# The opening block of a linear-attention and two-layer feed-forward kernel: the diagonal of y by products of its own, and another order of its queues

## The chip, the cores and the metric

The kernel runs on one core of one Trainium2 chip. The metric is device time in microseconds (us) for one execution, lower is better; a run's time is given as the median of several executions.

## The reference, cut to what matters

Four batches, eight heads, 768 tokens, 48 values a head. A linear attention with decay runs first, and two feed-forward layers follow it on the 3072 tokens.

```python
for t in range(S):                     # r, k, v: (4, 8, 768, 48), w, u: (8, 48)
    cur = einsum('bhd,bhe->bhde', u * k[t], v[t])
    y[t] = einsum('bhd,bhde->bhe', r[t], state + cur)
    state = w * state + einsum('bhd,bhe->bhde', k[t], v[t])
x = y as (B * S, H * D)                # 3072 x 384
x = relu(x @ w_in) ** 2 @ w_out        # 384 -> 2048 -> 384
x = (x @ w_a) * (x @ w_b) @ w_out2     # 384 -> 1536 -> 384
```

The term `cur` makes the diagonal: token t sees itself through sum over d of r, u and k, times v[t]. Everything earlier comes through the scores within a block of 64 tokens and through the state.

## The kernel before

**Tiles.** The tokens are cut into six blocks of 512, and a block into four units of 128 columns. A unit e holds 64 tokens of two batches (i = 0, 1), with the heads in pairs (g) of two (q). Per unit the attention does this: TensorE transposes k and r into PSUM (`turn_k`, `turn_r`), VectorE multiplies them with tables of powers of w into `kT` and `rT` (`scale_k`, `scale_r`), TensorE makes the scores (`score`, 32 small matmuls), VectorE copies the entries of earlier tokens into the `scores` tile through the mask `earlier` (`mask`), GpSimd and VectorE make the diagonal numbers `diag` (`k_times_u`, `times_r`, `sum_diagonal`), TensorE makes y from the state and the scores (`mix_state`, `mix_scores`) and the state's new part (`renew_state`), ScalarE copies y out (`take_y`) and VectorE the state (`keep_state`).

Before, the `scores` tile is first filled with a matrix that is zero apart from `diag` on its diagonal, and `mask` writes the rest over it. In the first block that matrix is made by eight ScalarE activations for units 0 and 2 (`make_diagonals`), by one VectorE multiplication for unit 1 (L1268) and by one GpSimd multiplication for unit 3 (L570).

**The feed-forward part.** Each product is made of three passes (hi x hi, hi x lo, lo x hi) over float32 split into two parts: `split_hi` (ScalarE, L383) and `split_lo` (VectorE, L389) split a tile of weights once; the token matrix `xT` is split as well. `up(n, f)` and `down(n, f)` are the first layer's step f in block n, 9 and 9 matmuls of 512 columns; `up2` and `down2` are the second layer's. The attention of block n + 1 is laid beside the steps of block n by the table `beside`.

**The opening.** Only the first block's attention has nothing to stand beside. It is written out by hand on each queue, and every queue runs strictly in the order written. `up(0, 0)` (L723) waits for all four units of x (`x_lo_made` 4). Units 0 and 1 get there through DMAs: `take_y` writes `y_pad`, `repack` on SyncE (SP, L359 and L361, six DMAs) brings it into `xT` rows, then `x_hi` (ScalarE, L935) and `x_lo` (VectorE, L1206). Units 2 and 3 get there by matmuls: `take_y` and `split_y`, `place_x` (L697, L698: 24 matmuls against one-hot matrices), `first_x_hi` and `first_x_lo` (L930, L1201).

SP's queue before: k and r of both halves, v of both halves (L348, two DMAs of 192 KB each half), then

```python
for i in range(2):
    load_weights(sp, i)
repack(sp, 0)
for i in range(2, STAGES + 1):
    load_weights(sp, i)
```

`load_weights(sp, i)` is three DMAs (L309, L310, L311) into slot i of `stage`; `split_hi(i)` waits for all three. `repack(sp, 0)` waits for `y_made` 2, the end of `take_y(1)`.

ScalarE's queue before: `u_rows`, `make_diagonals(0)`, `tail_pow` (L987), `take_y(0)`, `take_y(1)`, `make_diagonals(2)`, `split_hi(0)`, `split_hi(1)`, `take_y(2)`, `take_y(3)`, `x_hi(0)`, `x_hi(1)`, `first_x_hi(2)`, `first_x_hi(3)`, and so on.

VectorE begins with small memsets, a memset of 1152 columns (L1069), casts that build the one-hot matrices (L1071, L1075, L1077), and then the tables of powers (L1081 to L1099), for which `scale_k(0)` and GpSimd's first multiplication wait. GpSimd's own opening ends with a memset of 2176 columns (L514). `warm` and `warm_long` are matmuls whose result nobody reads.

## Time and the profile before

| | |
|---|---|
| median of 3 runs | 917.87 us (917.6 to 918.74) |
| the profiled execution's own time | 917.79 us |
| its span, first to last instruction | 916.0 us |
| TensorE matmul busy | 906.1 us, 99% |
| VectorE, ScalarE, GpSimd busy | 389.8, 285.9, 122.7 us |
| start of the first matmul of `up(0, 0)` | 29.41 us |

PE is TensorE's matmuls and PEld its weight loads, DVE is VectorE, ACT is ScalarE, POOL is GpSimd; a name with q (SPq, ACTq) is that engine's queue issuing a DMA. Times on a row count from the start of the span. A row of a timeline gives start, length, engine, line, operation, output <- input and how many; what stands in brackets is the idle time ahead of it and what ended it.

### The profile page before, as it was taken

To read this page: it belongs to the slowest core of one execution; us is meant where nothing else is said; L and a number is where in the kernel's file an instruction comes from. 1 tells how busy PE (TensorE), PEld (TensorE's weight loads), DVE (VectorE), ACT (ScalarE), POOL (GpSimd) and SP (SyncE) were. 2 spreads that over 40 slices of the span, in tenths; PEclk is the share of its full clock that TensorE was granted. 3 is DMA by queue.
4 is the path that set the end of the run, shared out by engine and by line. 5 is a ranking of instruction groups with operands and counts; after the bars stand their busy time and mean duration, and the time that the engine had idled before them with its cause. 6 is when DMAs were issued, how large, how long until landed. Compare 5 with 4: busy or idle time off the path is not lost.

```text
span 916.0 us, 16503 instructions
## 1 busy us (share of the span) xinstructions
PE 906.1 (99%) x6951; PEld 775.1 (85%) x6951; DVE 389.8 (43%) x600; ACT 285.9 (31%) x501; POOL 122.7 (13%) x125
## 2 busy tenths in 40 slices
PE   8999999999999999999999999999999999999997
PEld 6888888888888888888888888888888888888887
DVE  8778665546555555336542212322321222222122
ACT  3534433333333233345542222212222222222121
POOL 7355422232223221000000000000000000000000
PEclk9999999999999999999999999999999999999999
DMA  9987545636435320043330001002002002001001
GB/s 150 172 145 145 94 66 107 92 77 86 79 65 94 56 61 20 18 135 116 91 108 1 1 13 58 1 1 70 0 1 69 1 1 69 1 1 32 3 1 35
DMA packets 175736, 53.39 MB, mean 58 GB/s; under 512 B 147885, under 2 KB 174126, under 8 KB 175662
## 3 DMA queue, kind: packets, MB, share of 16 engines
q1 hardware_dynamic: 168640, 47.22, 25.6%
q10 hardware_dynamic: 7022, 5.12, 2.4%
q8 instruction: 55, 0.90, 0.4%
q14 instruction: 19, 0.16, 0.1%
HBM read 38.54 MB, written 9.44 MB: 52 GB/s over the span
## 4 chain that ended last, share of the span: by engine, by line
PE 96%; SPq 2%; DMA 0%; DVE 0%; issue 0%; ACT 0%
PE banks L853 11%; PE banks L855 11%; PE banks L854 11%; PE banks L739 8%; PE banks L723 7%; PE banks L740 7%; PE banks L743 7%; PE banks L725 7%; PE banks L724 7%; PE banks L867 5%; PE banks L871 5%; PE banks L868 5%; PE banks L641 1%; PE banks L654 1%; PE banks L621 1%; PE banks L664 1%
## 5 line engine op out<-in xcount | busy, mean ns | idle before, releaser
L1304 DVE TENSOR_TENSOR g_raw<-banks,g_raw 128x512 f32<-128x512 f32 x72 | 49.8, 692 | 277.0 <-PE banks L855 277.0
L853 PE MATMUL banks<-xT,weights 128*128 128x512 f32 x360 | 140.2, 389 | 0.0
L854 PE MATMUL banks<-xT,weights 128*128 128x512 f32 x360 | 140.0, 389 | 0.0
L855 PE MATMUL banks<-xT,weights 128*128 128x512 f32 x360 | 140.0, 389 | 0.0
L739 PE MATMUL banks<-g_hi,weights 128*128 128x512 f32 x288 | 114.8, 398 | 0.0
L723 PE MATMUL banks<-xT,weights 128*128 128x512 f32 x288 | 112.4, 390 | 0.8 <-DVE xT L1201 0.8
L1188 DVE TENSOR_TENSOR g_lo<-banks,g_hi 128x512 fp32r<-128x512 f32 x94 | 65.0, 692 | 112.7 <-ACT g_hi L915 112.7
L740 PE MATMUL banks<-g_hi,weights 128*128 128x512 f32 x288 | 112.2, 390 | 0.0
L724 PE MATMUL banks<-xT,weights 128*128 128x512 f32 x288 | 112.1, 389 | 0.0
L725 PE MATMUL banks<-xT,weights 128*128 128x512 f32 x288 | 112.0, 389 | 0.0
L915 ACT ACTIVATE g_hi<-banks 128x512 fp32r<-128x512 f32 x94 | 56.3, 599 | 148.3 <-PE banks L743 109.0
L1015 ACT ACTIVATE g_raw<-banks 128x512 f32<-128x512 f32 x72 | 43.1, 598 | 168.7 <-PE banks L855 168.7
L1018 ACT ACTIVATE g_hi<-g_raw 128x512 fp32r<-128x512 f32 x72 | 45.5, 632 | 160.6 <-DVE g_raw L1304 160.6
L1183 DVE TENSOR_TENSOR banks<-banks,g_raw 128x512 f32<-128x512 f32 x94 | 65.4, 696 | 51.0 <-ACT g_raw L909 50.7
L909 ACT ACTIVATE g_raw<-banks 128x512 f32<-128x512 f32 x96 | 57.3, 597 | 83.7 <-PE banks L725 83.6
L867 PE MATMUL banks<-weights,g_hi 128*128 128x384 f32 x240 | 80.9, 337 | 0.0
L743 PE MATMUL banks<-g_lo,weights 128*128 128x512 f32 x288 | 80.9, 389 | 0.0
L868 PE MATMUL banks<-weights,g_hi 128*128 128x384 f32 x240 | 80.6, 336 | 0.0
L855 PEld LDWEIGHTS banks<-xT,weights 128*128 128x128 f32 x360 | 67.5, 188 | 14.2
L853 PEld LDWEIGHTS banks<-xT,weights 128*128 128x128 f32 x360 | 67.6, 188 | 11.7
L854 PEld LDWEIGHTS banks<-xT,weights 128*128 128x128 f32 x360 | 67.6, 188 | 11.7
L1307 DVE TENSOR_TENSOR g_lo<-g_raw,g_hi 128x512 fp32r<-128x512 f32 x72 | 49.9, 693 | 50.2 <-ACT g_hi L1018 50.2
(131 smaller groups left out, 1247.8 us busy)
## 6 DMA issues: line engine op xcount, KB each, us to landing
rkv<-in_v SPq DMA_DIRECT2D x24, 192.0 KB, 4.5
x_dram<-stage SPq DMA_DIRECT2D x6, 768.0 KB, 3.5
xT<-x_dram SPq DMA_DIRECT2D x6, 768.0 KB, 5.4
result<-stage SPq DMA_DIRECT2D x22, 192.0 KB, 3.0
xT<-y_pad SPq DMA_DIRECT2D x22, 144.0 KB, 2.8
stage<-in_moe_w_out SPq DMA_DIRECT2D x16, 192.0 KB, 3.4
rkv<-in_k SPq DMA_DIRECT2D x12, 192.0 KB, 3.6
rkv<-in_k SPq DMA_DIRECT2D x24, 96.0 KB, 3.6
```

Source lines behind the costliest of these rows:

```text
L723: nc.tensor.matmul(hid[f % 2][:, :], hi, xT[:, q, HI, kt, :], start=(kt == 0), stop=False)
L724: nc.tensor.matmul(hid[f % 2][:, :], hi, xT[:, q, LO, kt, :], start=False, stop=False)
L725: last = nc.tensor.matmul(hid[f % 2][:, :], lo, xT[:, q, HI, kt, :], start=False, stop=(kt == KT - 1))
L739: nc.tensor.matmul(acc[m][:, :], hi(m), g_hi[:, f % 2, :], start=(f == 0), stop=False)
L740: nc.tensor.matmul(acc[m][:, :], lo(m), g_hi[:, f % 2, :], start=False, stop=False)
L743: last = nc.tensor.matmul(acc[m][:, :], hi(m), g_lo[:, f % 2, :], start=False, stop=(f == N1 - 1))
L853: nc.tensor.matmul(dst, hi, xT[:, q, HI, kt, :], start=(kt == 0), stop=False)
L854: nc.tensor.matmul(dst, hi, xT[:, q, LO, kt, :], start=False, stop=False)
L855: last = nc.tensor.matmul(dst, lo, xT[:, q, HI, kt, :], start=False, stop=(kt == KT - 1))
L867: nc.tensor.matmul(acc2[b][:, 0:DM], p_hi, hi, start=(j == 0), stop=False)
L868: nc.tensor.matmul(acc2[b][:, 0:DM], p_hi, lo, start=False, stop=False)
L1183: nc.vector.tensor_tensor(squared(n, f), squared(n, f), g_raw[:, f % 2, :], ALU.mult)\
```

## The change

For units 0 to 3 alone:

- **The diagonal.** The tiles of scores are zeroed once and get no diagonal. Instead v is multiplied with `diag` (`vd_of`: VectorE's `times_diagonal` for units 0, 2 and 3, eight ScalarE activations for unit 1), and 32 more matmuls of TensorE (`mix_diagonal`) add v times diag, through the 64x64 identity `eye`, to y. `make_diagonals`, L1268 and L570 are gone. One memset of 1024 columns is new on VectorE, ahead of its memset L1069.
- **Banks.** y of units 2 and 3 lies in banks (4, 5) and (6, 7), so `mix_state` needn't wait for the masks; their new states lie in banks 4 and 7, and `place_x` writes banks 0 to 3, with one matmul of 384 columns and three of 128 in place of six of 128 for each of its four parts.
- **States.** The states of units 0 and 1 are copied by ScalarE (`first_state`) and not by VectorE; those of units 2 and 3 are added in two halves.
- **Orders.** SP issues `repack(0)` ahead of the weights of step 1. `mix_diagonal(0)`, `score(2)`, `mix_diagonal(1)` and `score(3)` stand ahead of `renew_state(0)` on TensorE, the `warm_long` of L823 is gone, GpSimd's order is another, and `x_lo(0)` is on GpSimd.
- **v, in every block.** The second batches' heads are loaded swapped, in two DMAs of 96 KB and not one of 192 KB, so each half takes three DMAs.

```diff
@@ sync queue
-            for i in range(2):
-                load_weights(sp, i)
+            load_weights(sp, 0)
             repack(sp, 0)
-            for i in range(2, STAGES + 1):
+            for i in range(1, STAGES + 1):
                 load_weights(sp, i)
...
         def load_v(eng, e):
-            for i in range(2):
-                eng.dma_start(v_of_half(e)[i * T:(i + 1) * T], heads(v, e, i)).then_inc(v_loaded[e // 2 % 2], 16)
+            load_tokens(eng, e, v_of_half(e), v, v_loaded)
@@ gpsimd
-            for e in range(2, UNITS):
-                k_times_u(e)
+            k_times_u(2)
             pool.wait_ge(tail_made, 1)
             tail(0)
-            for e in range(2, UNITS):
-                times_r(e)
+            times_r(2)
             tail(1)
-
-            pool.wait_ge(tail_turned, 1)
-            pool.wait_ge(diag_made, UNITS)
-            nc.gpsimd.tensor_tensor(scores_of(3), *matrix_of(3), ALU.mult).then_inc(odd_diagonals, 1)
+            k_times_u(3)
+            times_r(3)
             tail(2)
             tail(3)
+            pool.wait_ge(diag_made, UNITS)
             decay(2)
+            x_lo(pool, 0)
             decay(3)
@@ tensor
+            def mix_diagonal(e):
+
+                pe.wait_ge(vd_made[e % 2], e // 2 + 1)
+                for g in range(PAIRS):
+                    for q, i in QUARTERS:
+                        rows = slice(i * T, (i + 1) * T)
+                        last = nc.tensor.matmul(y(e, g, q, i, D), vd_of(e)[rows, 2 * g + q, :], eye[rows, :],
+                                                start=False, stop=(g == PAIRS - 1), skip_group_check=True)
                 last.then_inc(y_mixed, 1)
...
                     pe.wait_ge(made, count)
+                    y = y_part(y_in, e)
+                    to = placed(e, part)
+                    nc.tensor.matmul(to, choose_own[0:PR], y[:, 0:KT, :], start=True, stop=False)
                     for kt in range(KT):
-                        to, y = placed(e, part)[:, kt, :], y_part(y_in, e)
-                        nc.tensor.matmul(to, choose_own[0:PR], y[:, kt, :], start=True, stop=False)
-                        last = nc.tensor.matmul(to, choose_last[kt][0:PR], y[:, KT, :], start=False, stop=True)
+                        last = nc.tensor.matmul(to[:, kt, :], choose_last[kt][0:PR], y[:, KT, :], start=False,
+                                                stop=(kt == KT - 1))
...
             first_scores(0)
             first_scores(1)
+            mix_diagonal(0)
+            score(2)
+            mix_diagonal(1)
+            score(3)
 
             pe.wait_ge(y_made, 1)
             renew_state(0)
-            score(2)
-            score(3)
             pe.wait_ge(y_made, 2)
             renew_state(1)
-
-            pe.wait_ge(state_made, 1)
-            warm_long(bank[5])
             mix_state(2)
             mix_state(3)
             first_scores(2)
             first_scores(3)
+            mix_diagonal(2)
+            mix_diagonal(3)
@@ scalar
+            def first_state(e):
+                act.wait_ge(mixed, e + 1)
+                nc.scalar.activation(state[0:PR, e % 2 * 2:e % 2 * 2 + 2, :, :].rearrange("p i g d -> p i (g d)"),
+                                     both(y_banks(e), PAIRS * T, PAIRS * D)[0:PR], ACT.Copy).then_inc(state_made, 1)
+
-            act.wait_ge(masks_made, 6)
-            make_diagonals(0)
             act.wait_ge(tail_turned, 1)
             nc.scalar.activation(tail_pow[:, :, :], bank[3][:, :].rearrange("p (h d) -> p h d", h=H)[:, :, 0:D],
                                  ACT.Copy).then_inc(tail_made, 1)
-            take_y(0)
-            take_y(1)
-            make_diagonals(2)
+            half_loaded(act, v_loaded, 1)
+            act.wait_ge(diag_made, 2)
+            for h in range(H):
+                last = nc.scalar.activation(vd_of(1)[:, h, :], v_heads(1)[:, h, :], ACT.Copy,
+                                            scale=diag[:, 1, h // 2, h % 2:h % 2 + 1])
+            last.then_inc(vd_made[1], 1)
+            for e in range(2):
+                take_y(e)
+            for e in range(2):
+                first_state(e)
             for i in range(2):
                 split_hi(act, i)
             take_y(2)
@@ vector
             nc.vector.memset(ones_row, 1.0).then_inc(rows_set, 1)
+            nc.vector.memset(scores[:, :, :, :, :], 0.0).then_inc(scores_zeroed, 1)
...
             dve.wait_ge(masks_made, 6)
             sum_diagonal(0)
-            sum_diagonal(1)
-            dve.wait_ge(diag_made, 2)
-            nc.vector.tensor_tensor(scores_of(1), *matrix_of(1), ALU.mult).then_inc(odd_diagonals, 1)
             mask(0)
             mask(1)
+            sum_diagonal(1)
             for e in range(2, UNITS):
                 scale_k(e)
+            times_diagonal(0)
             for e in range(2, UNITS):
                 scale_r(e)
             sum_diagonal(2)
-            keep_state(0)
+            mask(2)
+            times_diagonal(2)
+            mask(3)
             sum_diagonal(3)
-            keep_state(1)
-            mask(2)
-            mask(3)
+            times_diagonal(3)
             split_lo(nc.vector, 0)
             for e in range(2, UNITS):
                 split_y(e)
-            for e in range(2):
-                x_lo(e)
             for e in range(2, UNITS):
                 first_x_lo(e)
+            x_lo(nc.vector, 1)
             split_lo(nc.vector, 1)
             keep_state(2)
```

## Rows read from the trace of the kernel before

**Rows 1.** The page: busy time by engine, and the chain that ended last.
```profile
PE 906.1 (99%) x6951; PEld 775.1 (85%) x6951; DVE 389.8 (43%) x600; ACT 285.9 (31%) x501; POOL 122.7 (13%) x125
...
PE 96%; SPq 2%; DMA 0%; DVE 0%; issue 0%; ACT 0%
```

**Rows 2.** Windows: stretch, length, busy by engine, granted clock, DMA share, GB/s.
```profile
28.00:32.00 4.00, 3.16 (x63) 2.62 (x52) 3.55 (x6) 1.50 (x4) 1.23 (x1) 1.00 0.67 161
32.00:60.00 28.00, 28.00 (x280) 23.11 (x279) 20.31 (x29) 12.72 (x21) 12.88 (x12) 1.00 1.10 173
```

**Rows 3.** Chain that ended last, in order of time: start, us, what.
```profile
18.40 0.71 SPq L359
19.15 2.49 SPq L359
...
23.67 3.14 DMA xT<-y_pad
...
27.39 1.03 DVE xT L1206 x2
...
29.41 0.50 PE banks L723
```

**Rows 4.** Timeline of VectorE and GpSimd in the opening.
```profile
1.21 1.02 DVE L1069 MEMSET stage<- 128x1152 f32 x1 [0.19 <-issue]
...
2.27 0.46 DVE L1071 CAST xT<-stage 128x512 fp32r<-128x512 f32 x1
...
2.83 2.28 DVE L1075 CAST xT<-ident 128x48 fp32r<-128x48 f32 x2
...
3.16 1.91 POOL L514 MEMSET stage<- 128x2176 f32 x1
...
5.08 0.11 DVE L1081 COPY w_pow<-banks 128x8 f32<-128x8 f32 x1
...
12.87 1.04 POOL L557 TENSOR_TENSOR g_raw<-g_raw,w_pow 128x512 f32<-128x512 f32 x1
```

**Rows 5.** Timeline of TensorE, ScalarE and VectorE for units 0 to 3.
```profile
16.29 1.16 PE L654 MATMUL banks<-scores,rkv 64*64 64x64 f32 x64
...
17.05 1.08 ACT L926 ACTIVATE y_pad<-banks 112x512 f32<-112x512 f32 x2 [1.90 <-PE banks L654]
...
18.10 0.69 PE L621 MATMUL banks<-rT,kT 48*64 48x64 f32 x32
...
22.93 0.84 ACT L383 ACTIVATE weights<-stage 128x768 fp32r<-128x768 f32 x1 [1.13 <-DMA stage<-in_moe_w_out]
...
24.72 1.29 DVE L1196 TENSOR_TENSOR g_lo<-banks,g_hi 112x512 fp32r<-112x512 f32 x2 [0.82 <-ACT g_hi L926]
```

**Rows 6.** Timeline of TensorE: first and last of the 24 matmuls of place_x.
```profile
24.83 0.30 PE L697 MATMUL banks<-g_hi,xT 112*128 112x128 f32 x1 [0.34 <-ACT g_hi L926]
...
27.43 0.28 PE L698 MATMUL banks<-g_lo,xT 112*128 112x128 f32 x1
```

**Rows 7.** Timeline of SP's queue: weights of step 2, and a later repack.
```profile
25.99 0.43 SPq L311 DMA_DIRECT2D stage<-in_moe_w_out  x1
...
200.72 1.34 SPq L359 DMA_DIRECT2D xT<-y_pad  x2
202.10 2.51 SPq L361 DMA_DIRECT2D xT<-y_pad  x4
```

**Rows 8.** DMA issues, the one at 25.99: last number is us to landing.
```profile
stage<-in_moe_w_out SPq DMA_DIRECT2D x1, 192.0 KB, 2.6
```

**Rows 9.** Windows at the end of the span; columns as in the second group.
```profile
911.00:912.00 1.00, 0.35 (x2) 0.03 (x1) 0.56 (x1) 0.35 (x1) 0.00 (x0) 1.00 0.00 0
...
913.00:914.00 1.00, 0.00 (x0) 0.00 (x0) 0.00 (x0) 0.00 (x0) 0.00 (x0) 0.75 0.96 264
```

**Rows 10.** Transposes of L591, early and later: ns min/median/max, first and last start.
```profile
L591 PE MATMUL banks<-ident,rkv x16: 421/421/461, 6.3 to 9.8; 128*112 128x128 f32 x16
...
L591 PE MATMUL banks<-ident,rkv x16: 272/273/321, 12.7 to 16.1; 128*112 128x128 f32 x16
```

More of the change, by code:

```diff
@@ L54, in attention_ffn_kernel @@
     RKV = 2 * (2 * RK + DM) + HP - D
[L55 removed]
+    LOADS = 16 * 3
     B32 = 32
@@ L200, in placed @@
         def placed(e, part):
-            return bank[2 * e + part][:, 0:DM].rearrange("p (k t) -> p k t", k=KT)
+            return bank[2 * (e - 2) + part][:, 0:DM].rearrange("p (k t) -> p k t", k=KT)
         def matrix_of(e):
@@ L231, in attention_ffn_kernel @@
         diag_made, diagonals_set = sem("diag_made"), sem("diagonals_set")
-        even_diagonals, odd_diagonals = sem("even_diagonals"), sem("odd_diagonals")
+        vd_made, scores_zeroed = [sem(f"vd_made{i}") for i in range(2)], sem("scores_zeroed")
         y_mixed, mixed = sem("y_mixed"), sem("mixed")
@@ L651, in mix_scores @@
                     for q, i in QUARTERS:
-                        rows, h = slice(i * T, (i + 1) * T), 2 * g + (q ^ i)
+                        rows, h = slice(i * T, (i + 1) * T), 2 * g + q
                         v_head = v_flat(e)[rows, h * D:h * D + HP]
                         last = nc.tensor.matmul(y(e, g, q, i, HP), v_head, scores_of(e)[rows, q, g, :],
-                                                start=(e < 2 and g == 0), stop=True, skip_group_check=True)
+                                                start=(e < 2 and g == 0), stop=(e >= UNITS), skip_group_check=True)
+                if e >= UNITS:
+                    last.then_inc(y_mixed, 1)
+            def mix_diagonal(e):
[5 more added lines that the diff above has]
+                                                start=False, stop=(g == PAIRS - 1), skip_group_check=True)
                 last.then_inc(y_mixed, 1)
@@ L659, in renew_state @@
                 pe.wait_ge(k_tail_made, e + 1)
+                pair, at = state_place(e)
                 for g in range(PAIRS):
                     for q, i in QUARTERS:
-                        rows, h = slice(i * T, (i + 1) * T), 2 * g + (q ^ i)
-                        at = PAIRS * T + g * D
-                        last = nc.tensor.matmul(bank[banks_of(e)[i]][q * HP:q * HP + D, at:at + D],
+                        rows, h = slice(i * T, (i + 1) * T), 2 * g + q
+                        last = nc.tensor.matmul(bank[pair[i]][q * HP:q * HP + D, at + g * D:at + (g + 1) * D],
                                                 k_tail[rows, e % 2, 2 * g + q, :],
@@ L1171, in keep_state, with times_diagonal @@
                 to = state[0:PR, first_batch:first_batch + 2, :, :].rearrange("p i g d -> p i (g d)")
-                new = both(banks_of(e), PAIRS * T, PAIRS * D)[0:PR]
-                if e < 2:
-                    nc.vector.tensor_copy(to, new).then_inc(state_made, 1)
-                else:
-                    dve.wait_ge(decay_made, e - 1)
-                    nc.vector.tensor_tensor(to, new, decayed[0:PR].rearrange("p i g d -> p i (g d)"), ALU.add)\
-                        .then_inc(state_made, 1)
+                kept_part = decayed[0:PR].rearrange("p i g d -> p i (g d)")
+                pair, at = state_place(e)
+                dve.wait_ge(decay_made, e - 1)
+                if e < UNITS:
+                    for i in range(2):
+                        last = nc.vector.tensor_tensor(to[:, i, :], bank[pair[i]][0:PR, at:at + PAIRS * D],
+                                                       kept_part[:, i, :], ALU.add)
+                else:
+                    last = nc.vector.tensor_tensor(to, both(pair, at, PAIRS * D)[0:PR], kept_part, ALU.add)
+                last.then_inc(state_made, 1)
+            def times_diagonal(e):
+                half_loaded(dve, v_loaded, e)
+                dve.wait_ge(diag_made, e + 1)
+                if e >= 2:
+                    dve.wait_ge(y_mixed, 2)
+                nc.vector.tensor_tensor(vd_of(e), v_heads(e), diag[:, e % 2, :, :].rearrange("p g q -> p (g q)")
+                                        .unsqueeze(2).broadcast_to([P, H, D]), ALU.mult).then_inc(vd_made[e % 2], 1)
             def square(n, f):
@@ L1252, in layer1 @@
                     for e in beside[SPLIT].get(s, []):
-                        x_lo(e)
+                        x_lo(nc.vector, e)
                     if n == LAST and 8 <= f < 8 + KT:
```

59 lines of the change are left out of this document (30 added, 29 removed).

## The prediction

> **What bounds the kernel now.** I read the page first: TensorE is busy for 99% of the span and holds 96% of the chain that ended last [rows 1]. So only two things can move the time: TensorE's work after the opening, or the moment at which its unbroken work starts. The windows put that moment: busy for 3.16 of the 4 us from 28, then for 28.00 of 28 [rows 2]. The chain names it: the first matmul of `up(0, 0)` starts at 29.41 us, and the last waits behind it are SP issuing the repack from 18.40, its last DMA landing at 26.81 (23.67 + 3.14), `x_hi` on ScalarE, then VectorE's `x_lo` (1.03 for two) and `first_x_lo` [rows 3]. The reader should see that from 32 us on nothing idles, and that the time is 29.4 us of opening plus about 888 us of TensorE. The change leaves those 888 us as they are: the matmuls of blocks 1 to 5 are the same in number and shape. The third v DMA costs SP one more issue of some 0.65 us each half (a quiet repack's six take 3.85 [rows 7]); TensorE's unbroken work hides it [rows 2], so I cost it at nothing, and at 0.65 a half if that cover were gone. Everything is thus: when does `up(0, 0)` start, and at what clock?
>
> **Step 1, the tables.** VectorE's new memset has 1024 columns; by the row of 1152 columns in 1.02 us it takes 0.91 [rows 4]. It pushes the next memset's end from 2.23 to 3.1, and the cast L1071 then arrives while GpSimd's memset of 3.16 to 5.07 runs. The trace shows what that does: the second cast of L1075, issued before 3 us, ended only at 5.11, when that memset was over [rows 4]. So L1071 (0.46) and the casts behind it come after 5.07, and L1081 starts near 6.0 and not at 5.08: 0.9 late. The bounds are 0 (the cast slips in first and GpSimd's memset waits, for which nobody waits) and 1.3. The page SBUF — State Buffer of the Trainium skill ("SBUF: two separate sides") says that VectorE and GpSimd share one port pair by an exclusive lock, held for a whole instruction; by that rule the 0.9 is due, without it the sum would be 0.9 less; the trace agrees with the rule, with 2.28 us for casts of 48 columns.
>
> GpSimd and VectorE both start from these tables, and TensorE's `first_scores(0)` at 16.29 stands behind GpSimd's L557 (12.87 to 13.91), one run of transposes, a `warm_long` and eight more transposes. So all of it is 0.9 later. What was taken out (the ScalarE and VectorE diagonals) was not what `first_scores(0)` waited for: TensorE reached it at 16.29 straight from its own work.
>
> **Step 2, y of units 0 and 1.** Ahead of `take_y(1)` TensorE now has three more groups: `mix_diagonal(0)`, `score(2)`, `mix_diagonal(1)`. 64 mixing matmuls went in 1.16 us with the tail, so 32 cost 0.48; a score group starts the next after 0.59 (0.69 with its tail) [rows 5]. Sum 1.55. The eight activations of unit 1 took 2 us in their old form and are done before they are needed. `take_y(1)` ended at 18.13 (17.05 + 1.08) [rows 5]; it now ends at 18.13 + 0.9 + 1.55 = 20.6. Before, SP, busy with the weights of step 1, began the repack at 18.40 [rows 3], 0.3 us after y was there. So moving the repack ahead of them wins 0.3 us at most; the repack starts at 20.6 and not at 18.40.
>
> **Step 3, the repack's issues.** Before, the sixth issue started at 23.67, 5.27 after the first, and one of the six took 2.49 [rows 3]; with its own 0.6 that is 5.86 us; a quiet repack takes 3.89 (200.72 to 204.61) [rows 7]. With fewer transfers ahead I take 3.85, as most later ones: done at 24.45. The bound above is 5.86.
>
> **Step 4, the wait that takes the place of the old one.** The weights of step 1 are now issued behind the repack, from 24.45 on. ScalarE's queue is strict, and `split_hi(1)`, which needs all three of their DMAs, stands ahead of `take_y(2)`, `take_y(3)`, both `x_hi` and both `first_x_hi`. Before it waited 1.13 us, for a DMA issued ahead of the repack [rows 5]. The nearest row for the new place is the weights that stood behind the repack before: L311 issued at 25.99, 1.73 us after the repack's end at 24.26, landed 2.6 later [rows 7, 8]: 4.3 us from the end of the repack. With two quiet issues of 0.43 ahead of it, as long as its own, it is 0.9 + 2.6 = 3.5. I take 3.9: landing at 28.35. Queued behind the wait are y of units 2 and 3, which TensorE has ready near 24.5, and so `place_x`, `split_y` and `first_x_lo`. The repack's own landing (about 26) no longer matters.
>
> **Step 5, from that landing to `up(0, 0)`.** `split_hi(1)` 0.84 and `take_y(2)` 0.54 (half of the 1.08) [rows 5], with 0.25 for signals: `place_x(2)` starts 1.65 later. Its four parts cost, at 0.111 for 128 columns (24 of them in 2.6 us) [rows 6], 0.17 + 3 x 0.111 = 0.50 each against 0.67 (0.17, for 384 columns, is an estimate: three quarters of the 0.23 between matmuls of 512). VectorE's `split_y` (1.29 for two) keeps up, but for 0.15. The last part ends 3.8 after the landing, the last `first_x_lo` at 4.45, and `x_lo(1)` at 4.95 (0.5 each by the pair of 1.03) [rows 3]. `x_lo(0)` on GpSimd, 1.0 us, is done by then. So `up(0, 0)` starts 5.0 after the landing, at 33.35, which is 3.95 late. What `place_x` wins (4 x 0.17) is inside.
>
> **Step 6, the clock.** Between `mix_diagonal(3)`, about 24.5, and `place_x(2)`, about 30.0, TensorE has nothing to do for 5.5 us, where even the last 4 us before its unbroken work held 3.16 of matmuls [rows 2]; and one `warm_long` is gone. At the end of the span TensorE's last matmul ends at 911.35, and the granted clock falls in the window 913 to 914, whose mean of 0.75 is half at full and half at 0.50, the lower level of 1.2 GHz [rows 9]: some 2 us of idleness were enough there. So I expect the fall. Its price: the same transposes took 421 ns from 6.3 us and 273 from 12.7 [rows 10], and streamed work costs up to twice. `place_x`'s parts then go from 0.50 to about 0.95, back to back, which puts `up(0, 0)` 1.7 later; at the start the change to the faster form came between 9.8 and 12.7, with TensorE at work since 6.27, so after a resumption at 30.0 it should come near 36, and the first microseconds of `up` cost perhaps 0.8 more. Sum 2.5; bounds 0 (no fall) and 5 (the rise comes as late as 40). The page TensorE: Matmul & The Clock Gate ("What's actually happening") says that the throttled clock is the default and activity lifts it; the trace agrees at both ends. A rule that held the clock through such a gap would make it 2.5 less.
>
> **The sum.** 3.95 + 2.5 = 6.45 us on the profiled execution's own 917.79: 924.2. The median of the runs is 917.87, 0.08 above it, so the number stands.
>
> **Rivals.**
> *The clock holds.* The stall of step 4 comes, but TensorE stays at 2.4 GHz: 917.8 + 3.95 = 921.7; with both lower bounds of steps 1 and 4 (0 and 3.5) it is 920.4. For it speaks that one row is all I have of a fall, taken at the end of the span. Chance 0.20.
> *The weights are not late.* If the loads of step 1 landed within about 2 us of the repack, ScalarE would wait little, and the last wait would again be the repack: landing 20.6 + 3.25 + 2.4 = 26.25, plus the old 2.6 to the start of `up`: 28.85, or 0.6 us faster: 917.2, no change by measurement (0.2%, or 1.8 us, is about what tells from nothing). With step 1 at zero as well and the four small gains of `place_x` it is 1.9 to 2.2 faster: 915.8, and that is the case on the other side: it decides once `split_hi(1)` starts before about 25. No landing in the rows is that quick after a repack. Chances: 0.07 about equal, 0.08 faster.
> *More traffic than I think.* The repack keeps its 5.86 of issues and the clock rises late: 5.9 + 5 = 10.9, or 928.7. The v loads are the traffic that slowed it before, and they are over; chance 0.05.
> My forecast, stall and clock fall, has 0.60, with 922.5 to 927 as its own range.
>
> **How the numbers follow.** Faster by over 0.2%: 0.08. Within 0.2%: 0.08 (the equal case and the low edge of the second). Slower: 0.84. The range that leaves no more than 2 in 10 out runs from 919.8, just below the clock-holds rival at its lower bounds, to 928, just short of the heavy-traffic case.
>
> **What the profile would show.** Step 1: L1081 near 6.0 and GpSimd's first multiplication near 9.9. Step 2: the repack issued at 20 to 21, not near 18. Step 3: its six issues within 4 us. Step 4, the one on which all hangs: `split_hi(1)` idle for 4 to 6 us before it, released by the DMA `stage<-in_moe_w_out`, and `take_y(2)` at 29 or later. Step 6: a granted clock of 0.50 in a window around 29 to 35, and the first matmuls of L723 0.43 us apart and not 0.23. What would make me wrong: ScalarE not waiting there, or the chain of waits still running through the repack's landing.

## The result, and the profile after

| | before | after |
|---|---|---|
| median | 917.74 us (4 runs, 917.39 to 918.74) | 926.52 us (4 runs, 925.2 to 927.57) |
| the profiled execution's own time | 917.79 us | 926.34 us |
| its span | 916.0 us | 924.6 us |
| start of the first matmul of `up(0, 0)` | 29.41 us | 35.74 us |

The changed kernel is slower: ratio 1.0093, interval 1.0076 to 1.0111, some 8.6 us. The forecast was 924.2 within 919.8 to 928.0.

The page of the changed kernel, busy time and chain, against [rows 1]:

```profile
PE 908.0 (98%) x7069; PEld 778.1 (84%) x7069; DVE 391.2 (42%) x602; ACT 284.5 (31%) x495; POOL 122.8 (13%) x125
...
PE 97%; SPq 1%; DMA 0%; DVE 0%; issue 0%; ACT 0%
```

TensorE has 118 matmul records more and 1.9 us more of busy time; the span is 8.6 us longer. (The trace holds two records for each of the small float32 matmuls: the 64 calls of the four `mix_diagonal` are 128 of them.) So 6.7 of the 8.6 us are time in which TensorE did nothing; the added products (less the matmuls taken out), and what the lower clock cost it, lie within the 1.9.

The chain that ended last, in the opening (start, us, what), against [rows 3]:

```profile
20.46 0.61 ACT y_pad L962
...
21.08 0.71 SPq L374
...
24.42 0.59 SPq L376
...
25.05 1.39 SPq L322
...
26.49 0.46 SPq L323
...
26.99 2.99 DMA stage<-in_moe_w_out
...
30.00 0.84 ACT weights L398
...
31.48 0.41 PE banks L730
...
34.35 1.46 PE banks L697 x64
35.81 0.72 PE banks L758
```

Down to `place_x` this is the chain that the forecast named as the new one: `take_y(1)`, the repack's issues, then the three issues of step 1's weights and the landing of the last, `split_hi(1)` (L398), `take_y(2)` (L962), `place_x` (L730). The repack's own landing is no longer in it. Its end is another than the forecast's: not VectorE's `first_x_lo` and `x_lo(1)`, but TensorE's own `renew_state` of units 2 and 3 (L697).

ScalarE's timeline around it (start, us, engine, line, operation, tiles, and in brackets the idle time before it and what ended that), against [rows 5]:

```profile
30.00 0.84 ACT L398 ACTIVATE weights<-stage 128x768 fp32r<-128x768 f32 x1 [5.27 <-DMA stage<-in_moe_w_out]
30.75 1.07 ACT L962 ACTIVATE g_hi<-banks 112x512 fp32r<-112x512 f32 x2
```

The reader is to see the bracket: 5.27 us of idleness in front of `split_hi(1)`, where there were 1.13 before, and `take_y` of units 2 and 3 right behind it.

TensorE's timeline from the first score to the first matmuls of `up(0, 0)`:

```profile
11.86 0.70 PE L639 MATMUL banks<-rT,kT 48*64 48x64 f32 x32 [1.68 <-DVE rT L1168]
...
13.38 1.95 PE L609 MATMUL banks<-ident,rkv 128*112 128x128 f32 x8
...
16.90 1.04 PE L609 MATMUL banks<-ident,rkv 128*112 128x128 f32 x8
17.87 1.16 PE L676 MATMUL banks<-scores,rkv 64*64 64x64 f32 x64
...
22.75 0.70 PE L697 MATMUL banks<-rkv,k_tail 64*48 64x48 f32 x35 [1.54 <-issue]
23.71 1.11 PE L663 MATMUL banks<-rT,state 48*48 48x64 f32 x64 [0.26 <-ACT state L1015]
24.62 0.63 PE L676 MATMUL banks<-stage,rkv 64*64 64x64 f32 x27
27.41 0.82 PE L676 MATMUL banks<-stage,rkv 64*64 64x64 f32 x37 [2.16 <-issue]
28.02 1.10 PE L687 MATMUL banks<-eye,stage 64*48 64x64 f32 x64
31.48 0.41 PE L730 MATMUL banks<-g_hi,xT 112*128 112x384 f32 x1 [2.36 <-ACT g_hi L962]
...
35.74 0.79 PE L758 MATMUL banks<-xT,weights 128*128 128x512 f32 x1
```

Three things stand here. The wait in front of L730 on ScalarE's `g_hi` is the other side of the stall. Two waits marked "issue", 1.54 and 2.16 us, stand in the middle of groups of small matmuls, where nothing that the profile shows was waited for; 126 records (35, 64 and 27) lie between them, a number that comes back in experiments 5 and 6. And the first L609 group took 1.95 us where the same eight transposes took 1.04 three microseconds later.

For the last of the three the windows tell why (stretch, length, busy by engine, granted clock, DMA share, GB/s), against [rows 2]:

```profile
13.00:16.00 3.00, 3.00 (x32) 2.88 (x25) 3.00 (x6) 0.00 (x0) 2.73 (x3) 0.50 1.37 190
...
28.00:30.00 2.00, 1.12 (x80) 0.97 (x71) 0.00 (x0) 0.00 (x0) 0.00 (x0) 1.00 0.82 213
...
34.00:36.00 2.00, 2.00 (x67) 1.79 (x67) 1.61 (x3) 1.38 (x2) 0.00 (x0) 0.50 1.11 190
```

The granted clock was at its lower level of 1.2 GHz (0.50) twice, from 12.68 to 16.09 us, after TensorE had waited 1.68 us for `rT`, and from 33.16 to 36.57, after it had waited 2.36 us for ScalarE.

**Where the 8.55 us lie**, matmul by matmul against the trace before: +6.33 at the start of `up(0, 0)` (35.74 against 29.41), +0.37 over its first two matmuls, run at the lower clock, and then nothing until 75 us. There, in the middle of a plain `down` step, the timeline of TensorE has this:

```profile
74.52 0.51 PE L774 MATMUL banks<-g_hi,weights 128*128 128x512 f32 x1
...
76.45 0.50 PE L775 MATMUL banks<-g_hi,weights 128*128 128x512 f32 x1 [1.43 <-issue]
```

It is one gap, behind the small matmuls of the next block's attention, and it costs 1.7 us. The rest, 0.13 us, is spread. The page's own group for L775 shows that it is the only one of 288:

```profile
L775 PE MATMUL banks<-g_hi,weights 128*128 128x512 f32 x288 | 112.5, 391 | 1.4 <-issue 1.4
```

### The profile page after: what moved, and what is told of

Read it like the earlier page. It is cut to its first block, busy times and chain, and to the rows that moved or that the text cites. A ratio compares the mean times of both kernels' runs of the same rounds, so it can differ in the third digit from the quotient of the medians.

```text
span 924.6 us, 16750 instructions
## 1 busy us (share of the span) xinstructions
PE 908.0 (98%) x7069; PEld 778.1 (84%) x7069; DVE 391.2 (42%) x602; ACT 284.5 (31%) x495; POOL 122.8 (13%) x125
## 4 chain that ended last, share of the span: by engine, by line
PE 97%; SPq 1%; DMA 0%; DVE 0%; issue 0%; ACT 0%
PE banks L889 11%; PE banks L891 11%; PE banks L890 11%; PE banks L774 8%; PE banks L758 7%; PE banks L775 7%; PE banks L759 7%; PE banks L778 7%; PE banks L760 7%; PE banks L903 5%; PE banks L907 5%; PE banks L904 5%; PE banks L663 1%; PE banks L639 1%; PE banks L676 1%; PE banks L697 1%
## 5 line engine op out<-in xcount | busy, mean ns | idle before, releaser
L775 PE MATMUL banks<-g_hi,weights 128*128 128x512 f32 x288 | 112.5, 391 | 1.4 <-issue 1.4
```

The costliest lines, as they stand in the source:

```text
L775: nc.tensor.matmul(acc[m][:, :], lo(m), g_hi[:, f % 2, :], start=False, stop=False)
```

## The experiments

Six are edits of the changed kernel, or of it with an earlier edit in, and six of the kernel before; each is timed against the kernel before (917.4 to 918.2 in all of them). Gains and losses of the opening are given as the start of `up(0, 0)`, which was 29.41 before.

**1. The weights ahead of the repack again (on the changed kernel).**

```diff
-            load_weights(sp, 0)
+            for i in range(2):
+                load_weights(sp, i)
             repack(sp, 0)
-            for i in range(1, STAGES + 1):
+            for i in range(2, STAGES + 1):
                 load_weights(sp, i)
```

> The changed kernel with only SP's order undone: both weight loads ahead of the repack. Queue theory (ScalarE stood 5.27 us at split_hi(1) for weights issued behind the repack, and all of x behind it): the wait is gone, take_y(2) goes when y of unit 2 is ready, near 28.5, up(0,0) starts at 31.5 to 32.5 and not at 35.74, and the time falls by 3 to 4.5 us, to 922 to 923.5. Rival (the later tables and the added matmuls are the loss, and the order of the loads is harmless): less than 1 us back, 925.5 or more. Neither expects the 917.7 of the kernel before, since y of units 0 to 3 is still late.

Measured: 925.35 us (923.58 to 927.52), ratio 1.0085 [1.0068, 1.0103]; `up(0, 0)` at 34.35. The stall of `split_hi(1)` is gone, but only 1.4 us of the opening came back, where the expectation had 3.2 to 4.2. TensorE itself had become late. Its timeline in this run, and ScalarE's `take_y(2)`:

```profile
23.13 0.70 PE L698 MATMUL banks<-rkv,k_tail 64*48 64x48 f32 x35 [2.63 <-issue]
...
27.88 1.25 PE L677 MATMUL banks<-stage,rkv 64*64 64x64 f32 x35 [1.02 <-issue]
...
28.92 1.94 PE L688 MATMUL banks<-eye,stage 64*48 64x64 f32 x63
```

```profile
30.11 0.60 ACT L963 ACTIVATE g_hi<-banks 112x512 fp32r<-112x512 f32 x1 [4.26 <-PE banks L688]
```

Two "issue" gaps, and the clock at 0.50 from 23.84 to 30.66: the 63 records of `mix_diagonal` took 1.94 us, against 1.10 for 64 in the profile after. ScalarE now waits 4.26 us for y of unit 2, which is not there before 30 us, whatever ScalarE does. So the stall is not the only cause; a second one lies right under it.

**2. `split_hi(1)` behind `first_x_hi(3)` on ScalarE (on the changed kernel).** SP's new order stays; nothing stands behind the late weights.

```diff
-            for i in range(2):
-                split_hi(act, i)
+            split_hi(act, 0)
             take_y(2)
...
             first_x_hi(3)
-            for i in range(2, STAGES + 1):
+            for i in range(1, STAGES + 1):
                 split_hi(act, i)
```

> The changed kernel with SP's order as changed, but split_hi(1) moved on ScalarE's queue behind first_x_hi(3). Queue theory: the same weights land as late as before (near 30) and nobody stands behind them, so the time is within 0.7 us of the run with the weights first, 922 to 923.5. If instead late weights are dear in themselves (up(0,1) waits for their split), up(0,0) starts early but TensorE idles before up(0,1), and the time stays above 925.

Measured: 923.79 us (923.35 to 924.34), ratio 1.0068 [1.0053, 1.0083]; `up(0, 0)` at 33.34. That is 2.4 us of the opening and 2.7 of the median; the time is just above the expected range, and 1.6 and not 0.7 below run 1. The same two gaps (1.8 and 0.9 us) and a stretch at 0.50 from 23.41 to 30.24 stand in TensorE's way, and the gap near 75 us is there too (L775, 1.4 us).

**3. SP's new order alone, on the kernel before.** The edit is the first one turned round.

> The kernel before with nothing but SP's new order (repack ahead of the weights of step 1). Queue theory: repack issued from 18.2, done at 22.1 to 24.0, weights of step 1 landed at 26 to 28, take_y(2) after them at 27 to 29, and place_x with its old 2.7 us: up(0,0) at 31.5 to 33.5, slower by 2 to 4 us, and up to 2 more if the granted clock falls in the gap: 920 to 924. Rival (the order is harmless or wins 0.3 us, the loss sits in the rest of the change): 917.4 to 918.2.

Measured: 926.9 us (926.42 to 927.33), ratio 1.0099 [1.0083, 1.0116]; `up(0, 0)` at 36.60. The order of three issues alone costs what the whole change costs. ScalarE and TensorE in this run:

```profile
28.38 0.84 ACT L383 ACTIVATE weights<-stage 128x768 fp32r<-128x768 f32 x1 [6.58 <-DMA stage<-in_moe_w_out]
```

```profile
29.85 0.45 PE L696 MATMUL banks<-g_hi,xT 112*128 112x128 f32 x1 [5.46 <-ACT g_hi L925]
...
30.52 0.41 PE L697 MATMUL banks<-g_hi,xT 112*128 112x128 f32 x1
30.74 0.41 PE L696 MATMUL banks<-g_hi,xT 112*128 112x128 f32 x1
```

and one of its windows:

```profile
28.00:30.00 2.00, 0.15 (x1) 0.18 (x2) 0.26 (x1) 1.62 (x3) 0.00 (x0) 0.50 0.91 216
```

This is the forecast's steps 4 to 6 in the open, with 5.46 us of idle TensorE. The clock was at 0.50 from 27.03 to 40.69: `place_x`'s matmuls came 0.21 us apart where they were 0.11 apart before, and `up(0, 0)` ran its first nine or so 0.43 us apart. The expectation (up to 924) had less: ScalarE had the weights at 28.38 and not by 28, and it did not reckon with 13.7 us at the lower level.

**4. Three `warm_long` in the gap ahead of `place_x` (on the changed kernel).**

```diff
             mix_diagonal(3)
+            for _ in range(3):
+                warm_long(bank[0])
             pe.wait_ge(choice_made, 3)
```

> The changed kernel with three warm_long (six passes of 512 columns, 2.6 us, a result nobody reads) put between mix_diagonal(3) and place_x, where TensorE idled from 29.1 to 31.5. Clock theory: no window near 30 to 37 with a granted clock under 1.00, place_x and renew_state at full speed, up(0,0) near 34.3 and not 35.74, and 0.4 less after it: 1.2 to 2 us faster, 924.5 to 925.3. Rival (the half clock there costs nothing, since ScalarE and VectorE set the pace of place_x): within 0.5 us of 926.5. If the fall comes from the earlier stretch of idleness, the clock falls all the same.

Measured: 924.68 us (923.55 to 925.52), ratio 1.0076 [1.0061, 1.0091]; `up(0, 0)` at 35.71, so nothing of the opening came back. The clock fell in this run too, only earlier, at 23.25, before the unread matmuls had begun (29.48), and was back at 30.08. They also stood in the way themselves: behind them `place_x` started at 32.04, a microsecond after `take_y(2)` had y of unit 2 ready (30.9). The median lies in the expected range, but by luck: its 1.8 us came from elsewhere, there is no gap at 75 us here. The list of TensorE's waits has L697 and L676 for "issue", 1.5 and 1.0 us, and no L775. A kernel whose TensorE code is six records longer has lost that gap. So the edit says little about the clock, and a good deal about the gap: it depends on where in TensorE's code a matmul stands.

**5 and 6. Instructions or time? (on the kernel before).** If the "issue" gaps were only a matter of TensorE's extra work, 4 us of few long matmuls would do the same as 4 us of many short ones. Both are unread and stand behind the `warm_long` of L823. The short ones are 128 calls, 256 records, which is twice what the change adds, and the expectation is to be read with that.

```diff
+            def unread(n, small):
+                pe.wait_ge(masks_made, 6)
+                for j in range(n):
+                    if small:
+                        q, i = QUARTERS[j % 4]
+                        rows = slice(i * T, (i + 1) * T)
+                        nc.tensor.matmul(bank[4 + i][q * HP:q * HP + D, 0:T], eye[rows, 0:D],
+                                         eye[rows, :], start=True, stop=True)
+                    else:
+                        nc.tensor.matmul(bank[5][:, 0:T], ident[:, :], eye[:, :], start=True, stop=True)
...
             warm_long(bank[5])
+            unread(128, True)      # run 5; unread(18, False) in run 6
             mix_state(2)
```

> The kernel before with 128 small matmuls (64x48 against 64 columns, the form of mix_diagonal, the number that the change adds, a result nobody reads) behind warm_long of L823. Their own work is 1.9 us. Code theory (TensorE's gaps marked issue come where many small matmuls use up its instructions faster than the 16 KB pieces of code are loaded): besides the 1.9 us there is a new idle stretch of 1 us or more marked issue in this group or in the mixing behind it, up(0,0) starts 2.5 to 4 us late, 920 to 922. Rival (the count of instructions is free, only their busy time counts): no such stretch, up(0,0) 1 to 1.3 us late, 918.7 to 919.

> The kernel before with 18 matmuls of a whole 128x128 matrix against 64 columns in the same place, about the same 1.9 us of TensorE with a seventh of the instructions. Code theory: no new idle stretch marked issue, up(0,0) 1 to 1.3 us late, 918.7 to 919.2, at least 1 us faster than the run with 128 small ones. Rival: the same time as that run.

Measured: 925.77 us (925.18 to 926.4), ratio 1.0081 [1.0064, 1.0098], `up(0, 0)` at 36.73 with the many; 924.11 us (923.65 to 926.06), ratio 1.0068 [1.0053, 1.0083], `up(0, 0)` at 31.85 with the few. TensorE with the many short ones:

```profile
21.86 2.56 PE L777 MATMUL banks<-eye 64*48 64x64 f32 x154
26.69 1.61 PE L777 MATMUL banks<-eye 64*48 64x64 f32 x100 [2.27 <-issue]
...
30.54 0.79 PE L641 MATMUL banks<-rT,state 48*48 48x64 f32 x38 [1.84 <-issue]
```

and with the few long ones:

```profile
21.75 4.13 PE L780 MATMUL banks<-eye,ident 128*128 128x64 f32 x36
25.80 1.11 PE L641 MATMUL banks<-rT,state 48*48 48x64 f32 x64
```

2.56 + 1.61 = 4.17 us of short and 4.13 of long matmuls: the same time, but two gaps of 2.27 and 1.84 us for the one, none for the other (and for the one a stretch at 0.50 from 35.62 to 39.03, behind them). The opening loses 7.3 us against 2.4, both more than expected. In the whole time the two differ by only 1.7 us, since run 6 lost another 3.3 behind its opening and run 5 1.1. What TensorE runs out of is suggested by the DMA queues of the stretch 18 to 32 us, many and few (packets, MB, share of 16 engines):

```profile
q8 instruction: 4, 0.07, 1.7%
```

```profile
q8 instruction: 3, 0.05, 1.6%
```

Queue q8 brings pieces of code of some 16.4 KB. Over the whole span there were 55 in the kernel before, 56 in the changed one, 57 in run 5 and 55 in run 6, and TensorE's matmul records are 6951, 7069, 7207 and 6987: each piece goes with about 126 matmul records and their weight loads. 256 small matmul records in 4 us need two pieces where 36 long ones need a third of one. No row names the piece that an engine waits for, but two things in the kept traces do it. The first is the time. Here is when a packet of q8 landed, and when TensorE went on after an "issue" gap:

| | piece landed | TensorE went on |
|---|---|---|
| the changed kernel | 21.50, 26.07, 75.06 | 22.75, 27.41, 76.45 |
| run 1 | 21.66, 26.55, 73.50 | 23.13, 27.88, 74.74 |
| run 5 | 25.29, 29.11 | 26.69, 30.54 |

In all traces, 24 "issue" gaps of over 0.45 us stand later than 12 us, and each of them ends 1.2 to 1.6 us after a packet of q8 has landed. The second is the place. In the changed kernel and runs 1, 2, 8 and 9 the gaps stand behind 346, 472 and 1101 matmul records of TensorE, and in runs 4 and 7 behind 346 and 472, though run 7 has six more records ahead; the others stand behind 473 and 601 (run 5), 848 and 1351 (run 6) and 973 (run 11). Within three records, each of these lies a multiple of 126 behind 346. So the gaps are where a piece ends: TensorE stood waiting for the next.

Of what run 6 lost behind its opening, 2.2 us go to two gaps of the same kind (0.8 us each, ahead of 60.98 and 94.03; TensorE is 1.1 later behind each). Another 0.7 near 130 us is not of it: the profile puts the wait of 0.48 there to VectorE. The expectation, 918.7 to 919.2 us, had none of this.

**7. Six more `warm` at the start (on the changed kernel),** to see whether the early idleness costs.

```diff
-    WARM_START, WARM_TURNS = 8, 4
+    WARM_START, WARM_TURNS = 8, 10
```

> The changed kernel with 10 and not 4 warm transposes ahead of score(0), where TensorE idled 1.68 us. Two questions. (a) The gap of 1.4 us marked issue at 75.0 us (none in the run with three warm_long, which has as many more instructions): if it is a matter of where a piece of code ends, it is gone here too, and the distance from up(0,0) to the last matmul falls by 1.6 us. (b) The fall of the granted clock at 12.68 in the opening of the changed kernel: with the idle stretch cut to 1.0 us it doesn't come. The stall of ScalarE at split_hi(1) stays. Time 924 to 925.2; if neither holds, 926.5.

Measured: 924.81 us, ratio 1.0077 [1.005, 1.0105], with a wide spread: 928.68, 925.98, 922.97, 923.64. In the profile, the slowest of them, the fall at 12.68 us is gone and `mix_scores(0)` starts at 17.15 and not at 17.87, and the gap at 75 us is gone as well; but then:

```profile
32.28 0.66 PE L730 MATMUL banks<-g_hi,xT 112*128 112x384 f32 x1 [4.34 <-ACT g_hi L962]
```

TensorE was done earlier, waited 4.34 us for ScalarE and not 2.36, and the clock was at 0.50 from 31.03 to 41.27, through all of `place_x` and into `up`. Here the lower clock costs what the forecast's step 6 had (`up(0, 0)` at 37.74). The same kernel was 5.7 us faster in another execution, which has no trace, only its mean clock: 0.996 against 0.994. That is some 4 us less at the lower level, and work that runs at half the speed for 4 us loses 2. So the clock can be some 2 of the 5.7 us, and the rest stays open.

**8. The memset of `scores` on GpSimd (on run 2's kernel).**

```diff
             nc.gpsimd.memset(stage_words[:, STAGES * W2:], 0.0).then_inc(rest_zeroed, 1)
+            nc.gpsimd.memset(scores[:, :, :, :, :], 0.0).then_inc(scores_zeroed, 1)
...
-            nc.vector.memset(scores[:, :, :, :, :], 0.0).then_inc(scores_zeroed, 1)
```

> The changed kernel with split_hi(1) behind first_x_hi(3) (923.8 us in its own run), and besides the memset of the scores tile moved from VectorE to GpSimd, behind its last memset there. Tables theory: L1081's twin starts near 5.1 and not near 6.0, GpSimd's first multiplication at 9.0, take_y(1) ends 0.9 earlier, 922.5 to 923.2. Rival (the 0.9 is swallowed by waits behind it, code and clock): 923.5 to 924.2.

Measured: 924.45 us (922.39 to 926.44), ratio 1.0068 [1.0043, 1.0092]; `up(0, 0)` at 33.51, no gain. The four executions fall into two pairs, 926.44 and 926.36 at a mean clock of 0.994, 922.53 and 922.39 at 0.999; the trace is of the first pair, so the median says little. VectorE's timeline:

```profile
2.83 3.17 DVE L1114 CAST xT<-ident 128x48 fp32r<-128x48 f32 x2
...
5.97 0.11 DVE L1120 COPY w_pow<-banks 128x8 f32<-128x8 f32 x1
```

and GpSimd's:

```profile
5.01 0.95 POOL L535 MEMSET scores<- 128x1024 f32 x1
```

The pair of casts of 48 columns now lasts 3.17 us where it was 2.28 [rows 4]: it is held through both of GpSimd's memsets, and the tables start at 5.97 all the same, where 5.1 was expected. Later a gap of 1.7 us on TensorE near 73 was followed by a stretch at the lower clock, in the windows:

```profile
72.00:74.00 2.00, 0.41 (x1) 0.09 (x1) 1.28 (x2) 0.60 (x1) 0.55 (x1) 1.00 0.04 3
...
76.00:78.00 2.00, 2.00 (x6) 1.52 (x5) 0.13 (x1) 0.76 (x2) 1.37 (x2) 0.50 0.13 32
```

**9. The same memset on VectorE, behind `scale_r(1)` (on run 2's kernel).**

```diff
                 scale_r(e)
+            nc.vector.memset(scores[:, :, :, :, :], 0.0).then_inc(scores_zeroed, 1)
             dve.wait_ge(masks_made, 6)
...
-            nc.vector.memset(scores[:, :, :, :, :], 0.0).then_inc(scores_zeroed, 1)
```

> The changed kernel with split_hi(1) behind first_x_hi(3), and the memset of the scores tile on VectorE behind scale_r(1), where VectorE idled 0.58 us for GpSimd. Tables theory: the copy that starts the tables is back near 5.1, GpSimd's first multiplication near 9.0, TensorE's idle stretch ahead of score(0) is gone, take_y(1) ends 0.5 to 0.9 earlier than 20.3, and up(0,0) starts 0.5 to 0.9 before 33.3: 922.9 to 923.4. Rival (TensorE's supply of code takes the 0.9 back, since its gaps come where the small matmuls are, however early): up(0,0) within 0.3 us of 33.3, 923.5 to 924.2.

Measured: 922.99 us (922.38 to 923.14), ratio 1.0059 [1.0047, 1.0072], 0.8 less than run 2 (the ratios' intervals still overlap); `up(0, 0)` at 32.77, 0.57 earlier. The tables start at 5.08 as before, and the memset lies in a pause:

```profile
5.08 0.11 DVE L1119 COPY w_pow<-banks 128x8 f32<-128x8 f32 x1
...
11.62 0.91 DVE L1307 MEMSET scores<- 128x1024 f32 x1 [0.16 <-issue]
```

So step 1 was right in its price for the tables, and the memset's place was the cause.

**10. SP's new order with `split_hi(1)` moved (on the kernel before):** run 3 with run 2's edit.

> The kernel before with SP's new order (repack ahead of the weights of step 1) and split_hi(1) behind first_x_hi(3), nothing else. Queue theory: ScalarE no longer stands for those weights, the repack is out by 22 to 24 and landed by 24.5 to 26, and up(0,0) waits for place_x and renew_state instead: it starts at 28.5 to 29, and the time is 916.8 to 917.6, against 926.9 for the same order with split_hi(1) in its old place. If the late weights matter in themselves, TensorE idles ahead of up(0,1) and the time is 918 to 919.

Measured: 918.42 us (11 runs, 917.2 to 918.81), ratio 1.0008 [1.0, 1.0017]; `up(0, 0)` at 28.42, a microsecond earlier than before. Moving one instruction on ScalarE is worth 8.5 us against run 3. The microsecond won did not last, and the time is in the range of the expectation's second branch (918 to 919). TensorE and ScalarE:

```profile
34.41 0.47 PE L722 MATMUL banks<-xT,weights 128*128 128x512 f32 x1 [1.62 <-ACT g_raw L908]
```

```profile
31.29 0.85 ACT L383 ACTIVATE weights<-stage 128x768 fp32r<-128x768 f32 x1 [3.02 <-DMA stage<-in_moe_w_out]
32.94 0.84 ACT L383 ACTIVATE weights<-stage 128x768 fp32r<-128x768 f32 x1 [0.81 <-DMA stage<-in_moe_w_out]
```

The third matmul group, `up(0, 2)`, needs `read_relu(0, 0)` (L908), and that stands on ScalarE behind `split_hi(2)` and `split_hi(3)`, whose weights land later still.

**11. Run 10 with the wide `place_x` of the change:** one matmul of 384 columns and three of 128 a part, as the diff of the change has it.

> As the run above, with the change's place_x as well (one matmul of 384 columns and three of 128 for each of four parts, 16 matmuls for 24). If place_x is the last wait there, up(0,0) starts another 0.5 to 0.7 us earlier, 916.2 to 917.0. If the weights of step 1 are the last wait by then (up(0,1) at their split), nothing more is won. A piece of code may end elsewhere and cost or give 1 us in a later mixing.

Measured: 921.29 us (5 runs, 920.5 to 922.79), ratio 1.0047 [1.0033, 1.006]; `up(0, 0)` at 27.95. `place_x` itself won 0.47 us, and the wait ahead of `up(0, 2)` was 1.2 and not 1.6. The kernel is slower than run 10 by 2.9 us all the same, and its profiled execution (920.5) by 1.7. There TensorE has a gap at 70 us that run 10 doesn't have, and is 2.3 us later behind it. The waits of TensorE (total, times, longest):

```profile
PE banks L663 <- issue: 2.0, 1, 2.0
```

Its code has 8 matmul records fewer. Nothing in that gap waits for anything of `place_x`.

**12. A shorter tail of the opening (on the kernel before):** `x_lo(0)` on GpSimd, and `first_x_lo` ahead of `x_lo(1)` on VectorE.

```diff
             decay(2)
+            x_lo(nc.gpsimd, 0)
             decay(3)
...
-            for e in range(2):
-                x_lo(e)
             for e in range(2, UNITS):
                 first_x_lo(e)
+            x_lo(nc.vector, 1)
```

> The kernel before with one part of the change alone, the one that needs no TensorE instruction: x_lo(0) on GpSimd between decay(2) and decay(3), and VectorE's first_x_lo(2), first_x_lo(3) ahead of x_lo(1). Before, VectorE did four operations of 0.5 us behind the repack's landing at 26.81; two of them (the copies from PSUM) have their inputs by then, and one goes to GpSimd beside. Theory: up(0,0) starts 0.5 to 0.8 us before 29.41, nothing else moves since TensorE's code is the same to the instruction, and the time is 0.5 to 0.8 lower than before: 916.6 to 916.9. Rival: the weights of steps 1 and 2 or renew_state become the last wait (renew_state ended at 28.57), and less than 0.3 us is won.

Measured: 917.67 us (11 runs, 917.11 to 918.47), ratio 1.0001 [0.9992, 1.001]; `up(0, 0)` at 28.75, 0.66 earlier, and then:

```profile
33.78 0.47 PE L730 MATMUL banks<-xT,weights 128*128 128x512 f32 x1 [0.62 <-ACT g_raw L916]
```

The same wait as in run 10 takes all of it back. No version that ran beats the kernel before.

## Why the prediction was right, and where it was not

**What bounds the kernel.** Right for the opening. Wrong in one sentence: that the change leaves the 888 us behind the opening as they are, since blocks 1 to 5 have the same matmuls. They have, but those matmuls stand at another place in TensorE's code, and a gap of 1.43 us stood at 75 us that was not there before, behind which TensorE is 1.7 us later. Runs 4 and 7, each with six more matmul records ahead of it, lose that gap; runs 1, 2, 8 and 9, with as many as the changed kernel, keep it (1.0 to 1.7 us); run 11 shows one where run 10 has none. This 1.7 and the spread 0.13 are most of the 2.3 us by which the forecast was below the median (2.1 below the profiled execution).

**Step 1 (+0.9).** Right: L1121 at 5.90 against 6.0, GpSimd's first multiplication at 9.88 against 9.9. Runs 8 and 9 show the cause. Its rider was missed: TensorE's wait ahead of `score(0)` grew to 1.68 us, and the clock fell right behind it.

**Step 2 (repack at 20.6).** 21.08. The order of the terms was right; the half microsecond is the stretch at 0.50 from 12.68 to 16.09. Run 1, where all engines but SP have the same work up to here and the clock held, ends `take_y(1)` at 20.34 and not at 21.06: the stretch cost 0.7, and the forecast was 0.3 high without it.

**Step 3 (issues 3.85).** 3.93, from 21.08 to 25.01.

**Step 4, the stall.** Right in place and kind: 5.27 us ahead of `split_hi(1)`, released by the DMA of `stage<-in_moe_w_out`, `take_y(2)` at 30.75. The landing came 4.97 us after the repack's end and not 3.9, since the first of the three issues took 1.39 us on SP and the last landed 2.99 after its start. Together with step 2 this puts the landing at 29.98, 1.6 later than 28.35. Run 3 shows the mechanism alone, run 10 that it is the order on ScalarE that makes it cost.

**Steps 5 and 6 (5.0 from the landing to `up`, +2.5 for the clock).** The forecast ended step 5 on VectorE's `x_lo(1)`, and left out `renew_state` of units 2 and 3, which stands between `place_x` and `up` on TensorE. In the profile that is what `up(0, 0)` stood behind: `x_lo(1)` was done at 35.41, the 64 records of L697 at 35.81, since they took 1.53 us at 0.50 where they take 0.94 at 1.00 (run 1). Where the clock held (run 1) they were done first, and `up(0, 0)` waited 0.25 for `x_lo(1)`. From the landing to `up(0, 0)` it was 5.76 us, clock included, and 0.37 more over the next two matmuls. The clock has some 1.5 us of that and not 2.5: 0.6 in L697, 0.5 in the last part of `place_x` (1.09 us, the three before it 0.52 to 0.63), and the 0.37. What is left for step 5 is 4.6 or 4.7 and not 5.0. The clock fell later, 33.16 and not before `place_x`, for the reason in the timeline: I had TensorE idle for 5.5 us, but it was held up by two "issue" gaps of 1.54 and 2.16 us before, reached the end of `mix_diagonal(3)` at 29.1 and not at 24.5, and then waited only 2.36. In runs 3 and 7, where it did wait 5.46 and 4.34 us, the stretch at 0.50 was 13.7 and 10.2 us long and covered all of `place_x`.

**The sum.** 6.45 forecast, 6.70 measured once the first matmuls of `up(0, 0)` are through. That close a hit is partly luck: +1.6 in the landing, against 1.0 too much for the clock and 0.35 too much for step 5. And 0.7 of the 1.6 is a fall of the clock that the forecast did not have. The stall is also not alone in holding y of units 2 and 3 where the forecast has it: TensorE itself, by its gaps, had the last of it ready only at 29.1, and with the stall taken away (runs 1 and 2) 1.4 and 2.4 us of the opening came back, where the forecast's own rival without the stall has 4.5 (33.35 against 28.85).

**The rivals.** "The clock holds" is out, "the weights are not late" is out. "More traffic than I think" is out by the 3.93 us of step 3. None of the rivals had the cause that was missing: many small matmuls use up TensorE's code faster than it is brought. I had costed them by their time alone (0.48 us a group). Runs 5 and 6 show that at equal time their number decides: 7.3 us of the opening against 2.4. The landings and the counts of records there show that it is the code.

**How the causes overlap.** They don't add: SP's order alone costs 9.3 us (run 3 over its kernel before) in a kernel in which nothing else is late. In the changed kernel taking that stall away gives 2.7 back (run 2), because y of units 2 and 3 is late then by TensorE's own gaps and clock. Moving the memset gives 0.8 more (run 9). What remains, 5.5 us over the kernel before, goes to the diagonal's products, the other banks and copies, with their gaps (2.0, 1.1 and 1.4 us in run 9) and the clock. The kernel without `mix_diagonal` was not run, so how these 5.5 us split between the products' time, the gaps and the clock stays open. The mean clocks of the single executions don't settle it: run 4's only execution at 1.0 is its slowest (925.52), run 2's at 0.999 too (924.34), while in run 8 the two at 0.999 are 3.9 us faster. The gap at L697 was 2.6 us in run 1 and 1.5 in the profile after because TensorE reached it 0.7 us earlier there, and went on 0.4 later: its piece landed at 21.66 and not at 21.50, and TensorE took 0.2 longer from there.

## What to carry to other kernels

Before a load is put behind another transfer, look for the in-order queue that consumes it and for what stands behind the consumer there: here three issues moved cost 9.3 us, and moving the one consumer gave 8.5 back. Small matmuls are to be counted by number as well as by time, since each group of some 126 records needs another piece of code, and a gap behind it can open far from the edit; a difference of a microsecond or two between two versions with unlike instruction counts may be no more than that. And a gain in an opening is worth only what the next wait leaves of it: here `read_relu` behind `split_hi(2)` took back what runs 10 and 12 had won.

## What the runs showed of the hardware

- **Code comes in pieces.** Queue q8 moved 55 pieces for 6951 matmul records and 57 for 7207, 0.90 and 0.93 MB. Gaps of 0.9 to 2.6 us marked "issue" stand inside runs of small matmuls in every version with more of them in the opening, and single ones (1.0 to 2.0 us) near 70 to 75 us; they come and go with a few records more or less ahead of them. They end 1.2 to 1.6 us after a piece has landed, and lie multiples of some 126 matmul records apart.
- **The granted clock can fall after short idleness.** It did after 1.68 us (fall at 12.68 us in the changed kernel) and after the gap of 1.7 us at 73 us in run 8; it did not after the 2.16 us ahead of 27.41 in the changed kernel (1.00 in the window 28 to 30), so the length of one wait does not settle it. Stretches at 0.50 were 3.4, 6.8, 10.2 and 13.7 us long. In run 3 it stayed low while `place_x`, `renew_state` and the first matmuls of `up` ran without a pause.
- **A GpSimd memset holds VectorE's casts.** The memset reads nothing, and still casts of 48 columns lasted 2.28 us beside one memset and 3.17 beside two that followed each other: VectorE did not get in between them. The page SBUF — State Buffer of the Trainium skill ("SBUF: two separate sides") has the lock between VectorE's fast modes and GpSimd's operations; these runs agree, with a memset as the operation, though no row shows which mode a cast runs in.
- **SP's issues vary.** The first issue behind the repack took 1.39 us where the next took 0.46 and 0.43.
